# Attention and expert layer on one core: ninth block and small scores ahead of the product, scaling one step later, ScalarE's copy between its exponentials

## The reference

```
q_pool = q.reshape(B, H, S // 2, 2, D).mean(axis=3)      # 576 pooled queries a head
scores = scale * q_pool @ k.T                            # 576 x 1152
attn   = exp(scores - max(scores)); attn /= sum(attn) + 1e-9
x      = attn @ v                                        # heads side by side: 2304 x 512
h      = x @ w_in;  g = max(h, 0) + alpha * min(h, 0)    # 2304 x 2048
out    = g @ w_out                                       # 2304 x 512
```

## Time and profile before

| what | value |
|---|---|
| three runs | 993.22, 993.85, 993.98 us; median 993.85 |
| the profiled execution | 994.09 us, its span 991.4 us |
| PE busy | 894.2 us, 90% |
| DVE busy | 516.5 us, 52% |
| ACT busy | 417.6 us, 42% |
| POOL busy | 213.3 us, 22% |
| TensorE clock granted | 0.998 of full speed |
| DMA | 79.57 MB, mean 80 GB/s |
| row maximum, L432 | 144 of them, 1358 ns each |
| large exponential, L348 | 144, 1105 ns each |
| copies to `pt`: ACT L355, DVE L461 | 597 ns, 681 ns |

### The profile page before, as it was taken

The page is one execution under the profiler, slowest core; times in us unless marked ns, Lnnn a source line. Parts: engine busy times, 40 slices in busy tenths (PEclk is TensorE's granted clock), DMA queues, the critical chain, the costliest instruction groups (busy, mean ns, idle before and its releaser), DMA issues. The chain is left out here.

```text
span 991.4 us, 20910 instructions
## 1 busy us (share of the span) xinstructions
PE 894.2 (90%) x6896; PEld 625.5 (63%) x6896; DVE 516.5 (52%) x836; ACT 417.6 (42%) x963; POOL 213.3 (22%) x182
## 2 busy tenths in 40 slices
PE   3788888888888888888888889999999999999997
PEld 1444444444444444444444479999999999999996
DVE  2665665666666666656656644444444444444442
ACT  2555555555555555555555532222322222322222
POOL 2102111111211111121110032233333333332220
PEclk9999999999999999999999999999999999999999
DMA  7434423513533351342342011122142222422111
GB/s 175 117 83 105 106 67 77 124 48 78 123 88 83 77 124 48 77 124 73 80 96 67 1 55 64 63 63 64 56 126 63 63 64 63 128 64 63 63 42 64
DMA packets 36366, 79.57 MB, mean 80 GB/s; under 512 B 5360, under 2 KB 9456, under 8 KB 36336
## 3 DMA queue, kind: packets, MB, share of 16 engines
q1 hardware_dynamic: 33936, 74.48, 29.0%
q10 hardware_dynamic: 2400, 4.72, 1.4%
HBM read 74.46 MB, written 4.72 MB: 80 GB/s over the span
## 5 line engine op out<-in xcount | busy, mean ns | idle before, releaser
L432 DVE TENSOR_REDUCE neg_max<-s_ps 128x1 f32<-128x1152 f32 x144 | 195.5, 1358 | 20.9 <-DVEq L431 19.1
L355 ACT ACTIVATE pt<-slot_ps 128x512 f32<-128x512 f32 x144 | 86.0, 597 | 251.2 <-ACTq L354 251.2
L567 PE MATMUL pv_ps<-pt,v_f 128*64 128x256 f32 (+1 forms) x1152 | 170.1, 415 | 0.0
L581 PE MATMUL slot_ps<-ident,e_sb 64*128 64x64 f32 x2304 | 103.3, 228 | 72.3 <-PEq L576 72.3
L526 PE MATMUL s_ps<-k_f,q_f 64*128 64x512 f32 (+1 forms) x640 | 161.8, 625 | 5.0 <-PEq L537 5.0
L348 ACT ACTIVATE e_sb<-s_ps,neg_max 128x1024 f32<-128x1024 f32 x144 | 159.2, 1105 | 0.0
L581 PEld LDWEIGHTS slot_ps<-ident,e_sb 64*128 64x128 f32 x2304 | 87.6, 139 | 96.4 <-issue 96.4
L567 PEld LDWEIGHTS pv_ps<-pt,v_f 128*64 128x64 f32 x1152 | 73.8, 136 | 109.6 <-issue 81.5
L473 DVE COPY pt<-slot_ps 128x128 f32<-128x128 f32 x144 | 42.0, 292 | 174.0 <-DVEq L472 174.0
L610 PE MATMUL slot_ps<-x_hi,wi_hi 128*128 128x384 f32 x384 | 129.5, 337 | 1.1 <-PEq L606 1.1
L610 PE MATMUL slot_ps<-x_lo,wi_hi 128*128 128x384 f32 x384 | 129.5, 337 | 0.0
(11 more groups left out here) (46 smaller groups left out, 1046.4 us busy)
## 6 DMA issues: line engine op xcount, KB each, us to landing
q_raw<-in_q SPq DMA_DIRECT2D x64, 288.0 KB, 4.6
k_f<-in_k SPq DMA_DIRECT2D x64, 288.0 KB, 4.2
wi_raw<-in_w_in SPq DMA_DIRECT2D x48, 256.0 KB, 2.6
wo_raw<-in_w_out SPq DMA_DIRECT2D x48, 256.0 KB, 2.6
v_f<-in_v SPq DMA_DIRECT2D x32, 288.0 KB, 3.1
out<-pt ACTq DMA_DIRECT2D x6, 768.0 KB, 4.9
k_end<-in_k SPq DMA_DIRECT2D x64, 32.0 KB, 4.0
alpha_sb<-in_alpha SPq DMA_DIRECT2D x1, 8.0 KB, 4.7
```

The lines of the kernel that those rows point to most:

```text
L355: nc.scalar.activation(pt_half(t, 0), half_columns(slot_ps[0][:, :]), ACT.Copy).then_inc(slot_free[0], 1)
L432: nc.vector.tensor_reduce(out=neg_max[:, b:b + 1], in_=s_ps[:, S_AT[b]:S_AT[b] + NKEY], op=ALU.max, axis=AX_X, negate=True).then_inc(max_r ...
L567: ins = nc.tensor.matmul(pv_ps[h * D:(h + 1) * D, 0:n], v_f[2 * g + h][:, a, :], pt[:, a, at:at + n], start=(a == 0), stop=(a == KT - 1))
L581: ins = nc.tensor.transpose(slot_ps[i][:, a * HALF:(a + 1) * HALF], e_sb[rows, at:at + P], ident[rows, rows])
```

## The change

TensorE issues the ninth transpose and the small scores of s + 2 ahead of the product (and of the spreading) instead of behind it. ScalarE issues the small exponential of s + 1 ahead of its copy of slot 0, the large one behind it. VectorE computes the row maximum of s + 2 at the end of step s instead of that of s + 1 at its start, with one more of them ahead of the loop. The scalings move from the end of steps t = 8 and t = 4 to the start of steps t = 0 and t = 5; the last `scale(0)` stands behind the loop.

```diff
--- before.py
+++ after.py
@@ -351,10 +351,11 @@
 
             def step(s, pair, left=2):
                 t, g = s % TILES, s // TILES % 2
+                if left > 0:
+                    exponential_cut(s + 1)
                 act.wait_ge(tr_ready[0], 1).then_inc(tr_ready[0], -1)
                 nc.scalar.activation(pt_half(t, 0), half_columns(slot_ps[0][:, :]), ACT.Copy).then_inc(slot_free[0], 1)
                 if left > 0:
-                    exponential_cut(s + 1)
                     exponential(s + 1)
                 if t in SPREAD and (t == 6 or pair is not None):
                     n = GROUPS[SPREAD[t]][2]
@@ -455,22 +456,22 @@
 
             def step(s, pair, left=2):
                 t, g = s % TILES, s // TILES % 2
-                if left > 0:
-                    row_max(s + 1)
+                if t == 0 and pair is not None:
+                    dve.wait_ge(x_sb_free, 1).then_inc(x_sb_free, -1)
+                    scale(0)
+                if t == 5 and pair is not None:
+                    scale(1)
+                    dve.sem_inc(v_free[1 - g], 1)
                 dve.wait_ge(tr_ready[1], 1).then_inc(tr_ready[1], -1)
                 nc.vector.tensor_copy(pt_half(t, 1), half_columns(slot_ps[1][:, :])).then_inc(slot_free[1], 1)
                 if t in INVERT:
                     invert(INVERT[t])
                 if t == 5 and pair is not None:
                     x_high(pair + (0 if s < 2 * TILES else 1))
-                if t == 4 and s >= TILES:
-                    scale(1)
-                    dve.sem_inc(v_free[1 - g], 1)
-                if t == 8:
-                    dve.wait_ge(x_sb_free, 1).then_inc(x_sb_free, -1)
-                    scale(0)
                 dve.wait_ge(ninth_ready, 1).then_inc(ninth_ready, -1)
                 nc.vector.tensor_copy(pt_ninth(t), ninth_columns(t)).then_inc(slot_free[1], 1)
+                if left > 1:
+                    row_max(s + 2)
 
             def unit(f, h):
                 dve.wait_ge(h_ready, 1).then_inc(h_ready, -1)
@@ -493,8 +494,11 @@
                 dve.sem_inc(slot_free[i], 1)
             dve.sem_inc(pv_free, 1)
             row_max(0)
+            row_max(1)
             over_steps(dve, step)
             dve.wait_ge(alpha_in, 16).then_inc(alpha_in, -16)
+            dve.wait_ge(x_sb_free, 1).then_inc(x_sb_free, -1)
+            scale(0)
             for n in range(PASSES):
                 def hidden(f, i, first, last):
                     unit(f, 0)
@@ -586,19 +590,19 @@
                     begin_scores(s + 2)
                     for ins in big_scores(s + 2):
                         ins.then_inc(s_ready, 1)
+
+                pe.wait_ge(slot_free[1], 1).then_inc(slot_free[1], -1)
+                transposed(s, 2 * CH, NINTH).then_inc(ninth_ready, 1)
+                if left > 0:
+                    pe.wait_ge(exp_cut_done, 1).then_inc(exp_cut_done, -1)
+                if left > 1:
+                    small_scores(s + 2).then_inc(s_end_ready, 1)
                 group, tiles = PRODUCT[t]
                 if group == 0 or pair is not None:
                     if t in SPREAD:
                         pe.wait_ge(slot_free[0], 1).then_inc(slot_free[0], -1)
                         spread_inverse(SPREAD[t], slot_ps[0])
                     product(group, g if group == 0 else 1 - g, tiles)
-
-                pe.wait_ge(slot_free[1], 1).then_inc(slot_free[1], -1)
-                transposed(s, 2 * CH, NINTH).then_inc(ninth_ready, 1)
-                if left > 0:
-                    pe.wait_ge(exp_cut_done, 1).then_inc(exp_cut_done, -1)
-                if left > 1:
-                    small_scores(s + 2).then_inc(s_end_ready, 1)
 
             def hidden_unit(n, f, i, h):
                 if h == 0:
```

## The result

The changed kernel takes 960.92 us (median of four runs, 960.67 to 961.72) against 993.8 before: ratio 0.9672, 95% interval 0.9655 to 0.9688, 32.9 us faster. That lies in the range (935 to 965) and on the side forecast; the 949.0 was 12 us too good. The profiled execution took 960.71, its span 958.9.

The account below looks back on a forecast made before the run. TensorE, 90% busy, bounds the kernel, idling 66.3 us ahead of L581. Step by step a pair falls from 35.02 to 32.05: 2.97 times 15.1 pairs saves 44.9 us, giving 949.0 from 994.09 after 0.24 for the median; range 935 to 965.

Parts of the forecast that it names:

- (a): TensorE: ninth block and small scores go ahead of the product; L581 wait goes, stall about 0.15 a step replaces 0.36.
- (d): Scaling moved to the next step's start: VectorE's copy held until T + 1.04 at t = 0, T + 1.46 at t = 5.
- (b): VectorE's row maximum moved to the step's end: its copy no longer stands behind it, T + 0.87 instead of + 1.10.
- (c): ScalarE's small exponential ahead of its copy: copy slips from + 0.81 to about + 1.07, exponential loop 3.22 a step.
- The loop of 6.43 over two steps: VectorE copy and ninth, row maximum, exponentials, ScalarE copy, next but one transposes: 6.43 us, or 3.22 a step.
- the 13.58 at t3: Sum over one pair, row t3: next transposes start at 13.58, set by the exponential, against 13.48 by TensorE.
- t4's 16.71: Sum over one pair, row t4: next transposes start at 16.71, set by the exponential, against 16.34 by TensorE.
- the junction: TensorE, small scores followed by product, which no row showed: taken as 0.32, with 0.21 and 0.39 as ends.
- The end that I had put at 0.39: Upper end for small scores to product, 0.39 instead of 0.32: 10 us more, 959.
- the exponential loop's price of 961: Rival, chance 0.17: exponential loop ends last; if 0.3 a step longer, 12 us of the gain go: 961.
- that rival: Slower, chance 0.03: VectorE and ScalarE slow each other in PSUM, copy and reduction taking twice as long: 1040.

## Why the prediction was right, and where it was off
(a) TensorE's order: right in its timing to 0.02 (copy T + 0.86, ninth T + 1.70), and the wait at L581 went as said. The experiments add what the text did not say: without (d) this part loses 13 us, some 9 of it at the full clock.

(b) The row maximum was explained wrongly. The text has VectorE's copy freed from standing behind it by the move to the step's end. But the end of step s and the start of step s + 1 are the same place in VectorE's queue: ninth copy, row maximum, copy of slot 1 stand in this order in both kernels, as the earlier trace rows and the timeline of t = 7 above show. Only the scaling changed its place relative to them. The copy is earlier because the ninth and the small scores are, so the maximum starts while the product still runs. The number 0.87 was right, its reason belongs to (a).

(c) ScalarE's order: the small exponential's handover was put at 0.90, by likening it to the large one's 1.65. It is 0.59. The 1.65 held 0.3 of two further waits in TensorE's queue, shown by moving them (1.35). The loop of 6.43 over two steps was made with the 1.65, which holds in this order of the waits, and t = 4 (3.13 forecast and measured) confirms it where it ends last. In the sum, the 13.58 at t3 is not what the stated terms give (8.73 + 0.74 + 1.49 + 0.36 + 2.14 = 13.46): it allows 0.12 for the later small scores of t = 2 without saying so. The trace has 0.09 there (row maximum 0.83 behind the ninth of t = 2). The total does not hang on it, since t4's 16.71 starts from the ninth at 11.98. And s = 5 has a product, which the count of steps without one leaves out.

(d) The scaling: right (T + 0.61, wait 0.68 at the ninth of t = 5; 0.31 at t = 0).

**The term that was too small** is the junction, small scores to product: 0.32 taken, 0.39 measured. It counts in the six steps a pair whose end TensorE's own work sets and whose small scores have not the product's shape (t = 0, 1 and 5 to 8; t = 3 and t = 4 end by the exponential, in the forecast and in the trace): 0.42 of the 0.85 a pair. The overlap of 0.07 at a change of tile shape was right, and the small scores were longer: 0.46 (309.29) and not 0.39. The 0.39 came from a step in which TensorE reached them without having waited; where the ninth had waited for slot 1, they are 0.46 long, and such steps are what the change makes. Over the stage the mean of their records rose from 279 to 309 ns. The rows of the weight loads show one difference: in the earlier trace rows's step the load for the small scores starts together with the ninth transpose (328.10), in the same step of the changed kernel 0.12 behind it (309.26). The trace of before had a row of 0.46, right behind the ninth transpose of the earlier trace rows:
```profile
35.58 0.46 PE L514 MATMUL s_ps<-k_end,q_f 128*128 128x128 f32 x2
```
The sum should have taken it from there, as it took the stall of the ninth. The end that I had put at 0.39 was the value.
The second part is the 0.15 ahead of t = 2, slot 0 of the spreading step t = 1, missing from the sum and shown twice: the waits' order takes it to 0.31 or to nothing. Of the remaining 0.28, 0.14 is VectorE's copy at t = 6 (T + 1.01), with 0.23 of wait at the ninth; it is late in every second pair only, where the loop of 18 steps begins anew, and not at s = 132, where the steps written out follow the loop: the loop's jump is the likely reason, though nothing tried it. The rest is hundredths. 0.85 times 15.1 is 12.8 us, for the twelve missed.

The rule of the Trainium skill (TensorEngine Tiling (Array Packing), Key Properties: changing the tiling mode drains TensorE) agrees with the run of 64-row blocks: the product starts 0.12 earlier behind small scores of its own shape, and these start 0.08 later behind the ninth, where the change of shape now lies. Of the rivals, the exponential loop's price of 961 meets the time by accident: idle ahead of the transposes is 5.6 us, at t = 5 and t = 2 alone, the 320-column steps have none, and t = 2 to 4, where it had the loss begin, took 9.63 together against 9.68 forecast. VectorE and ScalarE hardly slow each other: VectorE's copy takes 692 ns in the mean where both run at once, 681 before, and the row maximum 1358 in both, where that rival needed twice as long.

## What to carry to other kernels
A reordering on one engine is worth what the other queues' order lets it be: of this change's parts, two cost 13 and 38 us alone (4 of the 13 by the clock) and all three together gain 33, so before a step is moved ahead of a long one, look for what its consumer's queue still does that waits for that long one. Where several waits stand ahead of an instruction, put the one that ends last at the end, step by step: each wait behind it cost 0.15 us here. And take the price of a junction from rows in which the engine had waited as it will in the new order, not from the steadiest ones.

## What the hardware showed that was not expected
- Three waits in TensorE's queue, in three orders, gave 960.9, 965.0 and 958.0 us. A wait passed after the last release costs 0.15 (1.65 and 1.35 from exponential to transposes with two and none behind it).
- The same small scores as two 128x64 matmuls take less than as one 128x128 where a 128x64 product follows: 0.50 from ninth to product against 0.54, and the product itself 1.18 against 1.23, with the same number of changes of tile shape.
- Small scores are 0.46 long behind a ninth transpose that waited and 0.39 behind one that did not.
- A wait can cost more than itself. In the two runs with TensorE's new order and the old scaling, the granted clock fell from 1.00 to 0.50 for some 3.5 us seven times, each time right behind a wait of 1.49, and the pair took 1.0 longer. In the other kernels, whose waits in this stage end at 1.3, every stretch of 5 us from 40 to 575 us shows 1.00.
